# Smaller first pieces for a dynamic convolution with a feed-forward block: two pieces of 512 tokens in place of one of 1024

## The reference

```python
w = exp(weight_gen - max(weight_gen, -1)); w = w / (sum(w, -1) + 1e-9)
x_pad = concatenate([zeros((B, 6, 192)), x], axis=1)
x_unf = x_pad[:, arange(S)[:, None] + arange(7)[None, :], :]   # (B, S, 7, 8 heads, 24)
out = einsum('bshk,bskhg->bshg', w, x_unf)                     # causal convolution, 7 taps
t = out.reshape(16384, 192)
h = t @ w_in
y = (h * sigmoid(1.702 * h)) @ w_out
```

## Time and profile before

| what | value |
|---|---|
| median of 3 runs | 1203.29 us (1198.86 to 1204.85) |
| the profiled execution: time, span | 1200.01 us, 1198.2 us |
| TensorE busy | 1140.1 us, 95% of the span, 9728 matmuls |
| VectorE, ScalarE busy | 793.6 us (66%), 572.1 us (48%) |
| transfers | 41.21 MB, mean 34 GB/s |
| mean granted TensorE clock | 0.992 of full speed |

### The profile page before, as it was taken

One profiled execution on the slowest core, in us unless ns is written; L12 is line 12 of the kernel. 1 busy time (PEld: TensorE's weight loads), 2 busy tenths in 40 slices (PEclk: granted clock), 3 DMA queues, 4 the chain that ended last, 5 costly groups with the idle time before them and its releaser, 6 DMA issues.

```text
span 1198.2 us, 21422 instructions
## 1 busy us (share of the span) xinstructions
PE 1140.1 (95%) x9728; PEld 920.3 (77%) x9728; DVE 793.6 (66%) x623; ACT 572.1 (48%) x594; POOL 0.2 (0%) x4
## 2 busy tenths in 40 slices
PE   0588999999999999999999999999999999999998
PEld 0476888888888888888888888888888888888886
DVE  8687585767749576674857658585775857676422
ACT  2356445454444444545445544544445454455443
POOL 0000000000000000000000000000000000000000
PEclk9989999999999999999999999999999999999999
DMA  6500100101010010101001010100101001010000
GB/s 209 196 1 1 63 1 9 55 1 64 1 63 1 1 63 1 63 1 63 2 1 63 1 63 1 41 24 1 63 1 63 1 21 44 1 63 1 27 1 27
DMA packets 7529, 41.21 MB, mean 34 GB/s; under 512 B 912, under 2 KB 1168, under 8 KB 5008
## 3 DMA queue, kind: packets, MB, share of 16 engines
q1 hardware_dynamic: 7440, 39.85, 9.9%
HBM read 24.12 MB, written 12.58 MB: 31 GB/s over the span
## 4 chain that ended last, share of the span: by engine, by line
PE 91%; DVE 6%; DMA 1%; ACT 1%; issue 1%; ACTq 0%; DVEq 0%
PE hid L345 43%; PE acc_main L363 29%; PE acc_rest L363 19%; DMA taps<-in_tap_runs 1%; DVE conv L256 1%; DVE prod L250 1%; DVE taps L268 1%; DVE tap_max L266 1%; DVE gate_lo L312 1%; ACT L201 0%; ACT gate L201 0%; ACT gate_hi L204 0%; DVE conv L250 0%; DVE w_lo L288 0%; DVE w L291 0%
## 5 line engine op out<-in xcount | busy, mean ns | idle before, releaser
L201 ACT ACTIVATE gate<-hid 128x1024 f32<-128x1024 f32 x256 | 263.2, 1028 | 554.2 <-PE hid L345 554.1
L312 DVE TENSOR_TENSOR gate_lo<-gate,gate_hi 128x1024 fp32r<-128x1024 f32 x256 | 312.5, 1221 | 316.7 <-ACT gate_hi L204 316.1
L345 PE MATMUL hid<-xt,w_hi 64*128 64x512 f32 x3072 | 444.9, 395 | 52.7 <-DVE xt L280 36.7
L345 PEld LDWEIGHTS hid<-xt,w_hi 64*128 64x128 f32 x3072 | 291.2, 187 | 123.3 <-DVE xt L280 36.7
L363 PE MATMUL acc_main<-gate_hi,w 64*128 64x512 f32 x2048 | 321.8, 392 | 0.0
L204 ACT ACTIVATE gate_hi<-hid 128x1024 fp32r<-128x1024 f32 x256 | 261.2, 1020 | 0.0
L363 PEld LDWEIGHTS acc_main<-gate_hi,w 64*128 64x128 f32 x2048 | 193.4, 186 | 45.7
L345 PE MATMUL hid<-xt,w_lo 64*128 64x512 f32 x1536 | 222.2, 395 | 0.0
L363 PE MATMUL acc_main<-gate_lo,w 64*128 64x512 f32 x1024 | 202.4, 392 | 0.0
L363 PE MATMUL acc_rest<-gate_lo,w 64*128 64x512 f32 x1024 | 202.2, 392 | 0.0
L363 PE MATMUL acc_rest<-gate_hi,w 64*128 64x512 f32 x1024 | 202.2, 392 | 0.0
(11 more groups left out here) (21 smaller groups left out, 119.3 us busy)
## 6 DMA issues: line engine op xcount, KB each, us to landing
xwin<-in_x_runs SPq DMA_DIRECT2D x16, 1056.0 KB, 5.6
out<-outs_main SPq DMA_DIRECT2D x16, 512.0 KB, 2.6
out<-outs_rest SPq DMA_DIRECT2D x16, 256.0 KB, 3.1
taps<-in_tap_runs SPq DMA_DIRECT2D x1, 3136.0 KB, 13.0
taps<-in_w_rows SPq DMA_DIRECT2D x2, 1536.0 KB, 10.5
w_hi<-w_hi SPq DMA_DIRECT2D x2, 768.0 KB, 7.2
w_lo<-w_lo SPq DMA_DIRECT2D x2, 768.0 KB, 7.2
taps<-in_tap_runs SPq DMA_DIRECT2D x2, 224.0 KB, 7.4
```

The lines of the kernel that those rows point to most:

```text
L201: nc.scalar.activation(gate[:, v % 2, :, :], hid[:, v % 2, :, :], ACT.Gelu_apprx_sigmoid).then_inc(gate_ready, 1)
L312: nc.vector.tensor_tensor(gate_lo[:, v % SLOTS, :, :], gate[:, v % 2, :, :], gate_hi[:, v % SLOTS, :, :], ALU.subtract).then_inc(gate_lo_r ...
L345: last = nc.tensor.matmul(hid[:, v % 2, h, :], w[rows, k, q, f], xt[rows, b, part, k, :], start=(i == 0), stop=(i == len(terms) - 1))
```

## The change

- The 256 positions of a run are cut into 17 pieces, `PIECES` = 8, 8 and fifteen times 16. The two narrow ones hold 512 tokens each.
- A narrow piece has 256 tokens on each half of the partitions. Its `xt` is written to columns 0 to 255, and four transfers (`spread`: rounded and remainder, either way) copy each half's columns to columns 256 to 511 of the other half, so that both halves have all 512 tokens. Then 8 units cover all features with the weights as they are loaded: the lower half takes the first half of the hidden width and the upper half the second. Matmuls have the shapes they had. The exchanged weights are first needed at unit 8 of piece 2.
- The output of a narrow piece is the sum of both accumulator halves with the columns exchanged, so its eviction has more and smaller steps.
- For piece 0, one copy each way is issued from SyncE's queue and one from ScalarE's. For piece 1 all four are SyncE's.
- `first_product` waits for the rounded part at its first matmul, for the remainder at the thirteenth, and for the remainder of `w_in` at the seventh, in units 0 and 2. That remainder is computed in two parts, 256 columns and then 768, with piece 0's remainder and the maxima of pieces 1 and 2 in between.
- Maxima and exponentials are taken piece by piece: pieces 0 to 2 at the start, piece j + 1 in units 0 and 2 of piece j after that (14 times). The piece's softmax steps follow in unit 3.
- Piece 1's convolution stands in units 0 to 4 of piece 0, and piece 2's begins in units 6 and 7 of piece 0 (7 steps) and ends in piece 1 (10 steps).
- The output in memory is (192, 16384), a row per channel, in place of 16 blocks of (192, 1024).

```diff
+NARROW, WIDE = 8, 16
+PIECES = (NARROW, NARROW) + 15 * (WIDE,)
-CONV_AT = (4, 0, 2, 1, 1, 2, 1, 1, 2, 1, 1, 1, 0, 0, 0, 0)
-TURN_AT, ROUND_AT, SPLIT_AT = 11, 12, 13
-TAPS_AT = (1, 3, 6, 8)
+MAX_AT, EXP_AT = 0, 2
+CONV_AT = ((5, 3, 3, 3, 3, 0, 0, 0), (1, 2, 2, 1, 2, 2, 0, 0), (0, 0, 0, 5, 2, 1, 2, 1, 2, 2, 1, 1, 0, 0, 0, 0))
+EARLY_AT = (0, 0, 0, 0, 0, 0, 5, 2)
+TURN_AT, ROUND_AT, SPLIT_AT = (5, 6, 11), (5, 6, 12), (5, 6, 13)
...
+        def spread(eng, j, part, to):
+
+            there, here = (LOWER, UPPER) if to == 0 else (UPPER, LOWER)
+            return eng.dma_start(xt[there, j % 2, part, :, HALF_N:N].bitcast(F32),
+                                 xt[here, j % 2, part, :, 0:HALF_N].bitcast(F32))
...
-            load_taps(1, 1, taps_loaded[1])
+            load_taps(1, 2, taps_loaded[1])
+            sp.dma_start(xwin[:, first_win:WIN, :], x_runs[:, first_win:WIN, :]).then_inc(x_added, 16)
+
+            sp.wait_ge(xt_hi_ready, 1)
+            spread(sp, 0, 0, 0).then_inc(xt_hi_spread, 16)
+            sp.wait_ge(xt_lo_ready, 1)
+            spread(sp, 0, 1, 0).then_inc(xt_lo_spread, 16)
+
             sp.wait_ge(w1_hi_ready, 1)
...
-            sp.wait_ge(w1_lo_ready, 1)
+            sp.wait_ge(w1_lo_ready, 2)
...
             sp.wait_ge(w2_lo_ready, 2)
-            load_taps(2, 1 + PARTS, taps_loaded[2])
+            load_taps(3, LAST, taps_loaded[2])
...
+            def load_window(j):
+                sp.wait_ge(conv_ready, j)
+                sp.dma_start(xwin[:], x_runs[:, START[j]:START[j] + WIN, :]).then_inc(x_reloaded, 16)
+
+
+            load_window(2)
+            sp.wait_ge(xt_hi_ready, 2)
+            for to in range(2):
+                spread(sp, 1, 0, to).then_inc(xt_hi_spread, 16)
+            sp.wait_ge(xt_lo_ready, 2)
+            for to in range(2):
+                spread(sp, 1, 1, to).then_inc(xt_lo_spread, 16)
+            store(0)
+            for j in range(1, LAST + 1):
+                if j + 2 <= LAST:
+                    load_window(j + 2)
+                store(j)
...
+            round_piece(0)
+            act.wait_ge(xt_hi_ready, 1)
+            spread(act, 0, 0, 1).then_inc(xt_hi_spread, 16)
+            act.wait_ge(xt_lo_ready, 1)
+            spread(act, 0, 1, 1).then_inc(xt_lo_spread, 16)
             exponentials(1)
+            exponentials(2)
...
             maxima_and_shift(0)
-            for q in range(CONV_STEPS):
-                conv_step(dve, 0, q)
-            turn_tile(0)
+            convolve(0, CONV_STEPS)
+            turn_piece(0)
             dve.wait_ge(w1_hi_ready, 1)
-            nc.vector.tensor_tensor(w1_lo[:, :, 0, :], w1_raw, w1_hi[:, :, 0, :], ALU.subtract).then_inc(w1_lo_ready, 1)
-            split_tile(0, 0)
+            w1_remainder(slice(0, 2 * P))
+            split_piece(0)
+            maxima_and_shift(1)
+            maxima_and_shift(2)
+            w1_remainder(slice(2 * P, FH))
             dve.wait_ge(w2_hi_ready, 1)
...
-            maxima_and_shift(1)
...
+                first, second = slice(0, HALF_N), slice(HALF_N, N)
+                dve.wait_ge(main_out_act, j + 1)
+                nc.vector.tensor_tensor(outs_main[:, 0, first], acc_main[:, 0, first], outs_main[:, 1, second], ALU.add)
+                nc.vector.tensor_tensor(outs_main[:, 0, second], acc_main[:, 0, second], outs_main[:, 1, first], ALU.add
+                                        ).then_inc(main_out_dve, 1)
                 for h in range(2):
-                    wait(dve, rest_crossed, 2 * j + h + 1)
+                    dve.wait_ge(rest_crossed, 2 * j + h + 1)
                     nc.vector.tensor_tensor(outs_rest[:, h, :], acc_rest[0:HALF, h, :], outs_rest[:, h, :], ALU.add
+                                            ).then_inc(rest_summed, 1)
+                dve.wait_ge(rest_summed, 2 * (j + 1))
+                for to, of in ((first, second), (second, first)):
+                    nc.vector.tensor_tensor(outs_rest[:, 0, to], outs_rest[:, 0, to], outs_rest[:, 1, of], ALU.add
                                             ).then_inc(rest_out, 1)
...
+                    if v == MAX_AT and j >= 2:
+                        maxima_and_shift(j + 1)
+                    convolve(j + 1, CONV_AT[kind(j)][v])
+                    if j == 0:
+                        convolve(2, EARLY_AT[v])
+                    if v == TURN_AT[kind(j)]:
+                        turn_piece(j + 1)
+                    if v == SPLIT_AT[kind(j)]:
+                        split_piece(j + 1)
...
+                    if v == 0 and i == 0:
+                        if is_narrow(j):
+                            pe.wait_ge(xt_hi_spread, 32 * (j + 1))
+                        else:
+                            pe.wait_ge(xt_hi_ready, j + 1)
+                    if v == 0 and i == 2 * SLICES:
+                        if is_narrow(j):
+                            pe.wait_ge(xt_lo_spread, 32 * (j + 1))
+                        else:
+                            pe.wait_ge(xt_lo_ready, j + 1)
+                    if n in (0, 2) and i == SLICES:
+                        pe.wait_ge(w1_lo_ready, 1 + n // 2)
```

More of the change, by code:

```diff
@@ L33, in ffn_of_dynamic_conv @@
     CB = x_runs.shape[2]
-    TILES = out.shape[0]
-    RUN = U * TILES
+    RUN = sum(PIECES)
     HALO = x_runs.shape[1] - RUN
@@ L42, in ffn_of_dynamic_conv @@
     REST = D - P
[L43 to L54, removed]
+    WIN = WIDE + HALO
+    N_CONV = WIDE * CB
+    HALF_N = N // 2
+    LAST = len(PIECES) - 1
+    START = [sum(PIECES[:j]) for j in range(len(PIECES) + 1)]
+    UNITS = [CH if u == WIDE else CH // 2 for u in PIECES]
+    UNIT0 = [sum(UNITS[:j]) for j in range(len(PIECES) + 1)]
+    NARROWS = [j for j, u in enumerate(PIECES) if u == NARROW]
+    assert N == 512 and CB == 32 * SLICES and REST == HALF and FH == CH // 2 * P and CH == 16 and NARROWS == [0, 1]
     with ExitStack() as ctx:
@@ L149, in _ @@
-            sp.wait_ge(w2_lo_ready, 2)
-            load_taps(2, 1 + PARTS, taps_loaded[2])
[L152 to L161, removed]
@@ L167, in _ @@
+            for j in range(1, LAST + 1):
+                if j + 2 <= LAST:
+                    load_window(j + 2)
+                store(j)
+            sp.wait_ge(main_stored, 16 * (LAST + 1))
+            sp.wait_ge(rest_stored, 16 * (LAST + 1))
         @block.scalar
         def _(act):
[L169 to L172, removed]
@@ L194, in lift @@
                     nc.scalar.activation(outs_rest[:, h, :], acc_rest[HALF:P, h, :], ACT.Copy).then_inc(rest_crossed, 1)
[L196 to L199, removed]
+            for j in range(LAST + 1):
+                for v in range(UNITS[j]):
+                    n = UNIT0[j] + v
+                    act.wait_ge(hid_ready, n + 1)
                     wait(act, gate_lo_ready, n - 1)
@@ L205, in tile @@
                                          ).then_inc(gate_hi_ready, 1)
-                    if v == EVICT_AT and not is_first(j):
+                    if v == EVICT_AT and j > 0:
                         lift(j - 1)
[L208 to L214, removed]
+                    if v == EXP_AT and 2 <= j < LAST:
+                        exponentials(j + 1)
+                    if v == ROUND_AT[kind(j)] and j < LAST:
+                        round_piece(j + 1)
+            lift(LAST)
         SOFTMAX_STEPS = 4
@@ L266, in maxima_and_shift, with convolve @@
                 nc.vector.tensor_reduce(most, t, AX_X, ALU.max).then_inc(taps_maxed, 1)
-                dve.wait_ge(taps_maxed, part + 1)
+                dve.wait_ge(taps_maxed, j + 1)
                 nc.vector.tensor_tensor(t, t, most.unsqueeze(2).broadcast_to(t.shape), ALU.subtract
                                         ).then_inc(taps_shifted, 1)
-            def turn_tile(j):
-                wait(dve, conv_ready, j + 1)
+            done = [0] * (LAST + 1)
+            def convolve(j, steps):
+                for q in range(done[j], done[j] + steps):
+                    conv_step(dve, j, q)
+                done[j] += steps
@@ L432 @@
         args.append(nc.dram_tensor(f"in_{name}", a.shape, _mybir.dt.from_np(a.dtype), kind="ExternalInput").ap())
-    args.append(nc.dram_tensor("out_0", (tiles, d, 2 * N), _mybir.dt.float32, kind="ExternalOutput").ap())
+    args.append(nc.dram_tensor("out_0", (d, b * s), _mybir.dt.float32, kind="ExternalOutput").ap())
     ffn_of_dynamic_conv(nc, *args)
     r = _run(nc, [arrays], core_ids=[0])
-    out = r.results[0]["out_0"].reshape(tiles, d, 2, U, LANES)
-    return _np.ascontiguousarray(out.transpose(2, 4, 0, 3, 1)).reshape(b * s, d)
+    pieces, out, at = r.results[0]["out_0"], _np.empty((2, LANES, run, d), x.dtype), 0
+    for u in PIECES:
+        cols = pieces[:, 2 * LANES * at:2 * LANES * (at + u)].reshape(d, 2, u, LANES)
+        out[:, :, at:at + u] = cols.transpose(1, 3, 2, 0)
+        at += u
+    return out.reshape(b * s, d)
```

222 lines of the change are left out of this document (119 added, 103 removed).

## The result

The changed kernel takes 1141.97 us in the median (1141.14 to 1143.88, 4 runs), beside 1201.12 us for the kernel before (4 runs). The ratio is 0.9507, with a 95% interval of 0.9475 to 0.9539: 59 us less, where 31.7 were forecast. The ratios of the experiments further down are to the kernel before as it ran beside each of them (1200.03 to 1203.1 us in the median).

A forecast was written before the change was run, and what follows sets the result against it. TensorE was taken as the bound, never waiting in the steady part, at 4.415 us a unit. Origin 22.9 + 3.2 = 26.1 against 57.8 gave 31.7 us less: 1203.3 - 31.7 = 1171.6, say 1171; range 1164 to 1184.

The forecast's parts named there:

- The start: Time until TensorE's first matmul: shorter piece 0 convolution, rounding, then copies of 3.9 us; about 24.4 us instead of 36.70.
- The bound from above, 5.7: Upper limit in us for piece 0's two side-by-side copies, should 1 KB descriptors go at a third of the pace.
- The first two units: Units 0 and 1 take 7.27 us at about half pace, against 8.83 in a steady rhythm.
- The origin before: Old kernel's unit start less 4.415 us for each unit before it: 1183.54 - 255 x 4.415 = 57.8 us.
- The 6.7 us of half-paced restarts: Part of the old 57.8 us, left for TensorE's slow restarts after its five waits for gate_hi.
- Unit 8: First unit of piece 1: its copies queue behind piece 2's window load; 0.5 us of stall, from 0 to 4.
- Rival A: Piece 0's copies slow, 5.7 us or more, or the window's load holds piece 1's back: 1179, to 1183; chance 0.12.
- The narrow evictions: Two narrow pieces' output evictions, in units 9 and 17, make second_product wait for the rest accumulator: 0.8 us each.
- Unit 16: First unit of piece 2: the late rounding costs 0.75 us and the remainder at the thirteenth matmul another 0.35, together 1.1.
- rival B: VectorE is the bound in the narrow pieces, with only 3.6 and 2 us to spare: 1176 to 1188; chance 0.12.
- The wide pieces: Added maxima, exponential and two table loads on each of 14 pieces stay within the slack: nothing.
- Rival C: Table changes are exposed in each of the 14 passes, 56 us added: 1227; decided from 2.3 us each; chance 0.03.

The follow-up runs named there:

- a_shift640: The changed kernel with tap_max at its old size, 224 columns instead of 64, so later tiles lie 640 bytes further; 1166.86 us, ratio 0.971 to the kernel before.
- b_moved: The kernel before with tap_max declared last and a 64-column filler in its place, so other tiles lie as after the change; 1173.55 us, ratio 0.9765.
- one_queue: The changed kernel with all four copies of piece 0 issued from SyncE's queue; 1140.72 us.
- filled: The changed kernel with four small softmax steps of piece 2 moved into VectorE's two gaps around piece 1's remainder; 1142.3 us.

## Why the prediction was wrong, point by point

**The step that failed** is in the first paragraph: "There are 256 units before and after the change, with the same 38 matmuls each", from which it follows that the steady 4.415 us stay and "the change is worth what it does to the origin". The number of matmuls stayed, their pace didn't: 226.7 ns a pair in place of 232.4, 27.7 us over the kernel. The cause, shown in both directions by a_shift640 and b_moved, is a line of the diff that I took for bookkeeping, the size of `tap_max`. No rival covered it, since all of them moved waits and none the pace. The 0.03 for a gain over 36 us had no mechanism behind it.

**The rest of the sum** can be held against a_shift640, which has the old pace. Its unit 255 starts at 1150.62. The forecast was 1183.54 - 31.7 = 1151.8, so the sum was 1.2 us off. By its terms, where a distance between unit starts says more than an idle time, since matmuls are slower just behind a wait:

- The start: 24.4 forecast, 23.57 measured. The convolution began 0.4 sooner than I had it. The copies took 3.88 us where I took 3.9, worked out from the copies of 768 KB. The bound from above, 5.7, was not needed: rows of 1 KB cost nothing extra that shows here.
- The first two units: 7.3 us, carried over from before. In a_shift640 unit 2 starts at 30.33, 6.8 us after the first matmul. This 0.5 and the 0.8 of the start add to 1.3, which is the difference.
- The origin before: the 119.63 taken for unit 14 is where the chain enters it. Its first matmul is at 119.47, which makes the old unit 4.4152 us and the origin 57.7 in place of 57.8. It moves nothing.
- The 6.7 us of half-paced restarts: gone with the waits. In the kernel before, the granted clock is 0.50 (1.2 GHz) from 56.6 to 66.8, with TensorE idle for the 7.3 us up to 61.45, and again from 77.1 to 80.4 and from 104.4 to 107.7. In the changed one it is 1.00 from 30 to 1129.
- The rule of the Trainium skill on several queues ("Trainium Kernel Development and Optimization", Key Constraints) is that transfers of all queues share the engines and that only issue time is saved. one_queue agrees with the first part: TensorE starts at 23.50 with one queue and at 23.57 with two. The issue time that it says is saved didn't show.
- Unit 8: 0.5 forecast, a wait of 0.3 measured. Rounded copies of piece 1 did end up behind the window's load, but only just late: in a_shift640 there is no wait, and units 2 to 8 take 0.1 more than six at the steady pace. Rival A didn't come.
- The narrow evictions: 0.8 each forecast, 0.4 of waiting each measured, 0.3 in a_shift640. By the unit starts there they cost 0.6 each.
- Unit 16: 1.1 forecast, 2.0 measured, 1.3 at the old pace in a_shift640 (1.9 by the starts of units 15 to 17). Here VectorE is the bound, as rival B had it, and a faster TensorE only arrives earlier. That gives back 0.7 of the pace's gain. By the starts in a_shift640 the four stalls add to 3.2 us, the number forecast, but made up otherwise: unit 8 and the evictions were put too high and unit 16 too low. That the sum came out is in part luck.
- The wide pieces: nothing forecast and nothing measured. TensorE's last wait is at 106, though ScalarE changes tables 30 times in place of 10. Rival C fails at its condition, no piece exposing any of its 2.3 us. The trace after shows the loads at 1283 ns, without the further 1.38 us that the Trainium skill ("ScalarE: Activation LUTs", What ACT_TABLE_LOAD costs) adds for a drain. The load at 109.49 ends at 110.77, and the gate behind it starts at 110.79.

```profile
109.49 1.28 ACT L244 ACT_TABLE_LOAD   x1
...
110.79 1.03 ACT L244 ACTIVATE gate<-hid 128x1024 f32<-128x1024 f32 x1
```

```profile
L208 ACT ACT_TABLE_LOAD x15 | 19.2, 1283 | 1.0 <-PEq L506 0.7
L244 ACT ACT_TABLE_LOAD x15 | 19.2, 1283 | 0.3
```

## What to carry to other kernels

Before you take an engine's steady pace as given, look for anything in the change that moves its operands, the size of a tile declared before them included: on a kernel whose TensorE is busy 97% of the span, 160 unused columns cost 24.9 us, 2.2%. If a matmul kernel's pairs are a few ns slower than a neighbour's, put a filler before the streamed operands and try steps of 64 bytes. When several things change at once, undo each alone, since the part that names the change may be the least of it. And time that one engine wins ahead of a step where it waits for another may only lengthen that wait, as in filled.

## What the runs showed of the hardware that was not expected

- The pace of float32r matmuls in row pairs (64 rows by 512 columns, two at a time) depends on the distance between weights and streamed operand: 226.7, 228.9, 232.4 and 233.3 ns a pair (386, 388, 391 and 393 ns for a matmul, since matmuls overlap) at 0, 64, 128 and 192 bytes more than the good distance, and 226.7 at 256 and when weights and operands moved by 128 together. These are the distances tried, in one layout, 64 and 192 in one run each, and the mechanism stays open. The weights moved by 128 alone gave 233.3, so the distance isn't all. Whether the common shift is free at other steps too wasn't tried.
- In the last 4 us of the changed kernel, when only second products are left, ten matmuls (five pairs) take 1.16 us where they took 1.13 just before, with the tiles in the good place. What makes them slower there is open:

```profile
1110.74 0.62 PE L444 MATMUL acc_main<-gate_hi,w 64*128 64x512 f32 x4
...
1111.87 0.84 PE L426 MATMUL hid<-xt,w_hi 64*128 64x512 f32 x6
...
1129.10 0.64 PE L444 MATMUL acc_main<-gate_hi,w 64*128 64x512 f32 x4
...
1130.26 0.64 PE L444 MATMUL acc_main<-gate_hi,w 64*128 64x512 f32 x4
```
